# RWKV attention and two MLP layers on one core: gate kept in PSUM, later diagonals, one load for r and k

## The chip, the cores and the metric

The kernel runs on one NeuronCore of one Trainium2 chip. The metric is the device time of one execution in microseconds (us); the median of three runs is 890.35 us. TensorE multiplies, ScalarE evaluates gates and rounds, VectorE and GpSimd do elementwise work, SyncE (SP) issues most DMAs.

## The reference

```python
for t in range(S):                       # B, H, S, D = 4, 8, 768, 48
    kt, vt, rt = k[:, :, t], v[:, :, t], r[:, :, t]
    cur = einsum('bhd,bhe->bhde', u[None] * kt, vt)
    y[:, :, t] = einsum('bhd,bhde->bhe', rt, state + cur)
    state = w[None, :, :, None] * state + einsum('bhd,bhe->bhde', kt, vt)
x = y as (B * S, 384)                    # 3072 tokens
h = x @ w_in; x = (h * sigmoid(1.702 * h)) @ w_out        # 384 -> 2048 -> 384
h = x @ w_in2; out = (h * tanh(softplus(h))) @ w_out2
```

## The kernel before, in words

The sequence is cut into 6 chunks of 128 steps. Chunk by chunk and batch by batch (24 blocks n; batch n % 4) attention is done with matmuls: the scores k·r of all pairs of steps of a chunk (`scores`, two PSUM banks), a mask (VectorE, `select`, line 741), the diagonal with u instead of the decay (`diagonal`: a reduction at 752 and a predicated copy at 757), the product with v (`inside`), the part from the state (`before`) and the new state (`update`, then `add_state`, 775 and 779). r and k are multiplied by powers of the decay first, by VectorE for the first blocks (`decay_half`, `decay_rk`) and by GpSimd later (`prepare`, 471); `bonus` (457, 459) is GpSimd's r*k*u for the diagonal. `decay_k` multiplies k in rows (735 on VectorE).

Each tile of the MLP is one chunk of all four batches, 512 columns. There are 6 tiles in each of the two layers. A tile has 16 units f, each 128 of the 2048 hidden features; in the first tile the first 10 units are done as two halves of 256 columns, so it has 26 steps. All numbers are split in a high part (rounded to TensorE's fp32r) and a low part, and each product is three: high*high, low*high, high*low. So a unit g is `up` (9 matmuls to a bank of h, line 1016), the gate, and `down` (9 matmuls into three accumulators, line 1045). There are 202 units in all and two banks of h. TensorE's order is written out by hand: step g issues up(g+2), with the attention work of the step behind its first matmul, and then down(g). What attention stands in which step is in the tables `SCORES` and `BURST` (first tile: scores of block 2 at step 1, its `inside` at step 3; block 3 at 4 and 6; 4 at 9 and 11; 5 at 12 and 14; 6 at 16 and 18; 7 at 19 and 21).

The gate is evaluated twice by ScalarE from the same bank: once to SBUF in full precision (`act1`, 589), once rounded to `g_hi` (592), which waits until down(g-2) has read the old `g_hi`. VectorE makes `g_lo = act1 - g_hi` (798). up(g) waits for `g_hi` of g-2, since its bank of h is free then. The weights' low parts in the first tile are made by GpSimd (482, 487).

y of a block is rounded to the high part of x by ScalarE (569), its low part is made by VectorE (764); for blocks of later tiles both go to a staging buffer `xt`, and SP moves them in 10 DMAs (`move_x`) to their place in x, `xs`. SP's queue is in the order of its code. r and k of a block come in two DMAs of 48 rows (48 or 64 in the first), to partitions 0 and 64.

At the start TensorE runs matmuls that nothing reads (`keep_warm`, 878; each call makes two instructions), turns the row u into columns (`selector_rows`, 963), and then goes to the scores of block 0. ScalarE copies those columns (617), then reverses the decay table (620), which VectorE needs for the second half of r and k.

The lines around the gate:

```python
act.activation(act1[:, g % 2, 0:c1 - c0], h_bank[g % 2][:, 0:c1 - c0], GATES[layer])
if g >= 2:
    act.wait_ge(g_used, g - 1)
act.activation(g_hi[:, g % 2, 0:c1 - c0], h_bank[g % 2][:, 0:c1 - c0], GATES[layer]).then_inc(g_done, 1)
```

Of the kernel before, what the change touches and what calls it, by code (L numbers as in the profile page):

```python
# [27 lines left out]
P = 128  # L28
CH = P
# [8 lines left out]
MOVES = 10  # L38
AHEAD = 2
BY_ACT = (0, 2)  # L40
WARM = (5, 10)
MID_STEPS = (3, 6, 9)
EARLY = 2
HALF = 10
# [10 lines left out]
def mlp_rwkv_program(nc, rk_d, r_d, k_d, v_d, w_d, u_d, wts_d, out_d):  # L55
# [9 lines left out]
    with ExitStack() as ctx:  # L65
        def sb(name, shape, dt=F32):
            return ctx.enter_context(nc.sbuf_tensor(name, shape, dt))

        def sem(name):
            return ctx.enter_context(nc.semaphore(name))  # L70
# [4 lines left out]
        wout_hi = sb("wout_hi", [P, NF, DM], F32R)  # L75
        wout_lo = sb("wout_lo", [P, NF, DM], F32R)
        xs = sb("xs", [P, 2, 2 * KD, TT], F32R)
        xt = sb("xt", [P, 2, HP, CH], F32R)
        mid = sb("mid", [P, NT * KD * TT])
        g_hi = sb("g_hi", [P, 2, TT], F32R)  # L80
        g_lo = sb("g_lo", [P, 2, TT], F32R)
        act1 = sb("act1", [P, 2, TT])


        ARENA = 9168
# [3 lines left out]
        def part(cols):  # L89
            place[0] += cols  # L90
            assert place[0] <= ARENA
            return arena[:, place[0] - cols:place[0]]
# [3 lines left out]
        mask = part(CH)  # L96
        ident = part(P)

        rk = [part(2 * HP * CH)[0:PR_ROWS, :].rearrange("p (a h t) -> p a h t", a=2, h=HP) for _ in range(2)]
        ks = [part(DM).rearrange("p (h d) -> p h d", h=H) for _ in range(2)]  # L100
        vs, rr = [part(DM).rearrange("p (h d) -> p h d", h=H)], [part(DM)]
        late = part(2 * DM)
# [30 lines left out]
        def first_operands(b):  # L133

            e = operands(b)
            if b == 0:
                e.amat = act1.rearrange("p a t -> p (a t)").rearrange("p (a h t) -> p a h t", a=2, h=HP)
            if b < EARLY:
                e.ks = held[b].rearrange("p (h d) -> p h d", h=H)
                e.vs = held[EARLY + b].rearrange("p (h d) -> p h d", h=H)  # L140
            return e
# [68 lines left out]
        win_ready, wout_ready = sem("win_ready"), sem("wout_ready")  # L210
        wout_first = sem("wout_first")
        h_done = sem("h_done")
        g_done = sem("g_done")
        glo_done = sem("glo_done")
        g_used = sem("g_used")
# [20 lines left out]

            return slot(f)[:, DM:2 * DM]

        def rk_rows(n):

            return ODD if n < EARLY else D

        def rk_half(n, j):

            rows = rk_d[bass.ds(n, 1)].rearrange("o j d a h t -> (o j d) a h t")
            return rows[D:2 * D] if j else rows[0:rk_rows(n)]

        def x_pieces(n):

            a, b = divmod(n, B)  # L250
            par = a % 2
            cols = slice(b * CH, (b + 1) * CH)
            for head in range(H):
                hp, half = divmod(head, 2)
                done = 0
                while done < D:
                    kd, q = divmod(head * D + done, P)
                    m = min(D - done, P - q)
                    q0 = hp % 2 * ODD + done
                    yield f32(xs[q:q + m, :, par * KD + kd, cols]), f32(xt[q0:q0 + m, :, half * 2 + hp // 2, :])  # L260
                    done += m

        def x_part(lo, par, kd):
# [9 lines left out]
        def x_block(lo, n):  # L273

            b = n % B
            if n < B:
                return xs[:, lo, 0:KD, b * CH:(b + 1) * CH]
            return xt[0:PR_ROWS, lo].rearrange("p (a i) t -> p a i t", a=2)

        def y_block(n):  # L280

# [53 lines left out]
        @block.sync  # L335
        def _(sp):
            def load_rk(n):
                sp.dma_start(buffers(n).rk[0:rk_rows(n)], rk_half(n, 0)).then_inc(rk_in[n % B], 16)
                if n >= EARLY:
                    sp.dma_start(buffers(n).rk[ODD:PR_ROWS], rk_half(n, 1)).then_inc(rk_in[n % B], 16)  # L340

            def load_k(n):
                sp.dma_start(buffers(n).ks, k_d[bass.ds(n, 1)].rearrange("o t h d -> t (o h) d")).then_inc(k_first[n] if n < EARLY else k_in[n % B], 16)
# [70 lines left out]
            for n in range(B, NT * B):  # L414
                if n + 2 < NT * B:
                    sp.wait_ge(y_done, n + 1)
                    load_rk(n + 2)
                move_x(n)
                if n + 2 < NT * B:
                    load_rest(n + 2)  # L420

            sp.wait_ge(xlo_done, NT * B)
# [14 lines left out]
        def _(pool):  # L437
# [28 lines left out]
            def prepare(n):  # L466

                a, b = divmod(n, B)
                e = buffers(n)
                pool.wait_ge(rk_in[b], a * 32 + 32)  # L470
                pool.tensor_tensor(e.rk, e.rk, decay, ALU.mult).then_inc(r_dec, 1)  # L471

            def rest(n):
# [69 lines left out]
        def _(act):  # L543
# [20 lines left out]
            def x_hi_part(n):  # L564

                act.wait_ge(y_done, n + 1)
                if n > B:
                    act.wait_ge(moved[(n - 1) % B], moves(n - 1))
                act.activation(x_block(0, n), y_block(n), ACT.Copy).then_inc(xhi_done, 1)

            def first_state(n):
# [11 lines left out]
            def gate(layer, g):  # L583

                f, c0, c1 = unit(g)
                act.wait_ge(h_done, g + 1)
                if g >= 2:
                    act.wait_ge(glo_done, g - 1)
                act.activation(act1[:, g % 2, 0:c1 - c0], h_bank[g % 2][:, 0:c1 - c0], GATES[layer])  # L589
                if g >= 2:  # L590
                    act.wait_ge(g_used, g - 1)
                act.activation(g_hi[:, g % 2, 0:c1 - c0], h_bank[g % 2][:, 0:c1 - c0], GATES[layer]).then_inc(g_done, 1)  # L592

            def copy_out(layer, t):

# [12 lines left out]
            act.wait_ge(cleared, 1)  # L608
            act.dma_start(powers[ODD:PR_ROWS, 0, 0, :], w_d[1]).then_inc(w_in, 16)
            act.dma_start(u_row, u_d).then_inc(u_first, 16)  # L610
            for n in range(EARLY):
                act.dma_start(first[n].rk[ODD:PR_ROWS], rk_half(n, 1)).then_inc(rk_in[n], 16)
            act.preload_act_table(GATES[0])
            act.wait_ge(cleared, 2)
            act.wait_ge(pick_rows, 1)
            for p0 in (0, ODD):
                act.activation(pick[p0:p0 + D, :], decay_bank[p0:p0 + D, 0:HP], ACT.Copy).then_inc(pick_copied, 1)

            act.wait_ge(runs, LOGS)
            act.activation(decay[:, 1], decay[:, 0, :, ::-1], ACT.Copy).then_inc(flipped, 1)  # L620
# [65 lines left out]
        def _(dve):  # L686
# [19 lines left out]

            def decay_half(n, a):

                dve.wait_ge(rk_in[n], 32)
                dve.tensor_tensor(first[n].rk[:, a], first[n].rk[:, a], decay[:, a], ALU.mult).then_inc(r_first, 1)  # L710

            def decay_rk(n):

                dve.wait_ge(rk_in[n], 32)
                dve.tensor_tensor(first[n].rk, first[n].rk, decay, ALU.mult).then_inc(r_first, 1)

            def split(win, wout):
# [63 lines left out]
            def attention(t, s):  # L781

                if s in SCORES[t]:
                    select(SCORES[t][s])
                    diagonal(SCORES[t][s])
                if s in BURST[t]:
                    x_lo_part(BURST[t][s])
                    if B <= BURST[t][s] < (NT - 1) * B:
                        add_state(BURST[t][s])

            def split_g(g):

                f, c0, c1 = unit(g)
                cols = slice(0, c1 - c0)
                dve.wait_ge(g_done, g + 1)
                if g >= 2:
                    dve.wait_ge(g_used, g - 1)
                dve.tensor_tensor(g_lo[:, g % 2, cols], act1[:, g % 2, cols], f32(g_hi[:, g % 2, cols]), ALU.subtract).then_inc(glo_done, 1)  # L798

            def split_mid(par, tile, kd):  # L800

# [65 lines left out]
        def _(pe):  # L867
# [89 lines left out]
            def selector_rows():  # L957

                pe.wait_ge(u_first, 16)
                for hp in range(HP):  # L960
                    for half, p0 in enumerate((0, ODD)):
                        d0 = (2 * hp + half) * D
                        ins = pe.matmul(decay_bank[p0:p0 + D, hp:hp + 1], u_row[:, d0:d0 + D], ident[0:1, 0:1], start=True, stop=True)
                ins.then_inc(pick_rows, 1)

            def early_sums(n):
# [26 lines left out]
            def up(g, beside):  # L993

                t, (f, c0, c1) = tile_of(g), unit(g)
                layer = t // NT
                par = t % 2
                hb = h_bank[g % 2][:, 0:c1 - c0]
                pe.wait_ge(win_ready, layer * NF + f + 1)
                if g >= 2:  # L1000
                    pe.wait_ge(g_done, g - 1)
                if f == 0 and layer:
                    pe.wait_ge(m_hi, (t - NT) * KD + KD)
                elif f == 0:
                    for b in range(c0 // CH, c1 // CH):
                        if t:
                            pe.wait_ge(moved[b], moves(t * B + b))
                        else:
                            pe.wait_ge(xhi_done, b + 1)
                for i, (w, lo) in enumerate(((win_hi, 0), (win_lo, 0), (win_hi, 1))):  # L1010
                    if f == 0 and lo and layer:
                        pe.wait_ge(m_lo, (t - NT) * KD + KD)
                    elif f == 0 and lo and t == 0:
                        pe.wait_ge(xlo_done, c1 // CH)
                    for kd in range(KD):
                        ins = pe.matmul(hb, w[:, f, kd, :], x_part(lo, par, kd)[:, c0:c1], start=i + kd == 0, stop=i == 2 and kd == KD - 1)  # L1016
                        if i == 2 and kd == KD - 1:
                            ins.then_inc(h_done, 1)
                        if i + kd == 0:
                            beside()  # L1020
# [105 lines left out]
```

## Time and profile before

| what | value |
|---|---|
| three runs | 889.5, 890.35, 891.91 us |
| the profiled execution | 891.0 us, its span 889.2 us |
| TensorE busy | 882.1 us, 99% |
| VectorE busy | 328.7 us, 37% |
| ScalarE busy | 292.5 us, 33% |
| GpSimd busy | 156.4 us, 18% |
| mean granted clock of TensorE | 0.998 of full speed |

Busy TensorE is time in which at least one matmul was in flight. The chain that ended last goes through TensorE for 96% of the span. In a timeline row, "x3" are three instructions run together, and what is in brackets is the engine's idle time before the first one and what released it.

### The profile page before, as it was taken

The page shows a single profiled execution, that of the slowest core. Times are in us where ns is not written, and L with a number is a line of the kernel's source. Part 1 is how long each engine was busy: PE and PEld are TensorE (multiplying, and loading weights), DVE is VectorE, ACT ScalarE, POOL GpSimd, SP SyncE. Part 2 cuts the span into 40 slices and gives each one's busy share as a digit, 9 for nine tenths or more (in the row PEclk, how much of TensorE's full clock was granted, in tenths as well). Part 3 has the DMA queues.
Part 4 walks back from the last instruction along what each step waited for, and adds up shares of the span by engine and source line. Part 5 has one row for each costly group of instructions (what it writes and reads, how often), then busy time and mean ns, then how long its engine had stood idle before and what let it go on. Part 6 is the DMA issues. An engine that isn't in the chain of part 4 may idle for free.

```text
span 889.2 us, 12953 instructions
## 1 busy us (share of the span) xinstructions
PE 882.1 (99%) x5168; PEld 730.6 (82%) x5168; DVE 328.7 (37%) x460; ACT 292.5 (33%) x540; POOL 156.4 (18%) x126
## 2 busy tenths in 40 slices
PE   9999999999999999999999999999999999999998
PEld 8998888887888878878888888888888888888886
DVE  6878336424443443543244222222222221221111
ACT  4542332232223222222454422322322322322322
POOL 5998403322231331120000000000000000000000
PEclk9999999999999999999999999999999999999999
DMA  9554303212330332221430000000000000000000
GB/s 248 170 170 118 95 25 97 83 48 63 88 99 12 86 93 63 51 77 38 157 107 18 1 0 1 36 1 1 35 1 1 36 1 1 35 1 1 36 1 35
DMA packets 37836, 49.54 MB, mean 56 GB/s; under 512 B 5873, under 2 KB 30322, under 8 KB 37778
## 3 DMA queue, kind: packets, MB, share of 16 engines
q1 hardware_dynamic: 37120, 48.13, 18.2%
q8 instruction: 42, 0.69, 0.3%
q10 hardware_dynamic: 658, 0.59, 0.3%
q14 instruction: 16, 0.13, 0.0%
HBM read 36.11 MB, written 4.72 MB: 46 GB/s over the span
## 4 chain that ended last, share of the span: by engine, by line
PE 96%; POOL 1%; DVE 1%; issue 1%; ACT 0%; POOLq 0%; DVEq 0%
PE h L1016 44%; PE acc L1045 43%; PE a_bank L895 2%; PE pair L928 2%; PE pair L941 1%; PE a_bank L953 1%; PE acc L878 1%; POOL win_lo L482 0%; POOL wout_lo L487 0%; DVE g_lo L798 0%; PE pair L878 0%; POOL arena L457 0%; PE h L895 0%; PE pair L914 0%; PE pair L921 0%
## 5 line engine op out<-in xcount | busy, mean ns | idle before, releaser
L798 DVE TENSOR_TENSOR g_lo<-act,g_hi 128x512 fp32r<-128x512 f32 (+1 forms) x202 | 173.1, 858 | 507.0 <-ACT g_hi L592 506.8
L1016 PE MATMUL h<-xs,win_hi 128*128 128x512 f32 (+1 forms) x1212 | 340.6, 384 | 0.2 <-POOL win_lo L482 0.2
L1016 PEld LDWEIGHTS h<-xs,win_hi 128*128 128x128 f32 x1212 | 220.2, 188 | 45.1 <-issue 0.7
L589 ACT ACTIVATE act<-h 128x512 f32<-128x512 f32 (+1 forms) x202 | 116.4, 576 | 268.9 <-PE h L1016 266.0
L592 ACT ACTIVATE g_hi<-h 128x512 fp32r<-128x512 f32 (+1 forms) x202 | 116.5, 577 | 254.4 <-PE acc L1045 254.3
L1045 PE MATMUL acc<-g_hi,wout_hi 128*128 128x512 f32 (+1 forms) x606 | 168.1, 379 | 0.0
L1045 PE MATMUL acc<-g_hi,wout_lo 128*128 128x512 f32 (+1 forms) x606 | 167.8, 379 | 0.0
L1045 PE MATMUL acc<-g_lo,wout_hi 128*128 128x512 f32 (+1 forms) x606 | 167.6, 378 | 0.0
L1016 PE MATMUL h<-xs,win_lo 128*128 128x512 f32 (+1 forms) x606 | 164.8, 380 | 0.0
L1045 PEld LDWEIGHTS acc<-g_hi,wout_hi 128*128 128x128 f32 x606 | 111.6, 189 | 21.8
L1016 PEld LDWEIGHTS h<-xs,win_lo 128*128 128x128 f32 x606 | 111.2, 188 | 22.0
L1045 PEld LDWEIGHTS acc<-g_hi,wout_lo 128*128 128x128 f32 x606 | 111.4, 189 | 21.3
L1045 PEld LDWEIGHTS acc<-g_lo,wout_hi 128*128 128x128 f32 x606 | 111.1, 188 | 21.3
L471 POOL TENSOR_TENSOR arena<-arena 112x1024 f32<-112x1024 f32 x20 | 48.7, 2437 | 129.7 <-DMA arena<-in_rk 129.7
L457 POOL TENSOR_TENSOR arena<-arena 128x384 f32<-128x384 f32 x22 | 24.4, 1110 | 99.0 <-DMA arena<-in_r 98.6
L757 DVE COPY_PREDICATED arena<-arena 128x1024 f32<-128x1024 uint32 x22 | 30.8, 1402 | 0.8
L895 PEld LDWEIGHTS a_bank<-arena 48*128 48x128 f32 x184 | 22.2, 187 | 8.1 <-issue 7.4
L895 PE MATMUL a_bank<-arena 48*128 48x128 f32 x184 | 26.4, 284 | 1.5 <-DVE arena L779 1.5
L895 PE MATMUL pair<-arena 48*128 48x128 f32 x184 | 26.5, 284 | 0.0
L606 ACT ACTIVATE mid<-acc 128x512 f32<-128x512 f32 x24 | 14.3, 598 | 33.8 <-PE acc L1045 33.8
L459 POOL TENSOR_TENSOR arena<-arena 128x384 f32<-128x384 f32 x22 | 23.4, 1063 | 1.7
L895 PEld LDWEIGHTS pair<-arena 48*128 48x128 f32 x184 | 22.2, 187 | 0.0
(92 smaller groups left out, 373.3 us busy)
## 6 DMA issues: line engine op xcount, KB each, us to landing
arena<-in_rk SPq DMA_DIRECT2D x44, 192.0 KB, 3.3
mid<-in_wts SPq DMA_DIRECT2D x16, 384.0 KB, 7.8
arena<-in_wts SPq DMA_DIRECT2D x16, 384.0 KB, 3.5
xs<-xt SPq DMA_DIRECT2D x117, 48.0 KB, 2.0
arena<-in_k SPq DMA_DIRECT2D x22, 192.0 KB, 2.6
arena<-in_r SPq DMA_DIRECT2D x22, 192.0 KB, 3.1
arena<-in_v SPq DMA_DIRECT2D x22, 192.0 KB, 2.7
out<-mid SPq DMA_DIRECT2D x5, 768.0 KB, 3.3
```

The lines of the kernel that those rows point to most:

```text
L457: pool.tensor_tensor(heads, heads, e.ks, ALU.mult).then_inc(rr_step, 1)
L459: pool.tensor_tensor(e.rr, e.rr, bonus_u, ALU.mult).then_inc(rr_step, 1)
L471: pool.tensor_tensor(e.rk, e.rk, decay, ALU.mult).then_inc(r_dec, 1)
L589: act.activation(act1[:, g % 2, 0:c1 - c0], h_bank[g % 2][:, 0:c1 - c0], GATES[layer])
L592: act.activation(g_hi[:, g % 2, 0:c1 - c0], h_bank[g % 2][:, 0:c1 - c0], GATES[layer]).then_inc(g_done, 1)
L606: act.activation(mid_cols(t - layer * NT, kd), acc[kd][:, :], ACT.Copy).then_inc(out_done[kd], 1)
L757: dve.copy_predicated(buffers(n).amat, ident.bitcast(mybir.dt.uint32).rearrange("p (a h t) -> p a h t", a=1, h=1).broadcast_to([P, 2, HP, ...
L798: dve.tensor_tensor(g_lo[:, g % 2, cols], act1[:, g % 2, cols], f32(g_hi[:, g % 2, cols]), ALU.subtract).then_inc(glo_done, 1)
L895: ins = pe.matmul(banks[half][:, hp * CH:(hp + 1) * CH], e.rk[p0:p0 + D, 1, hp, :], e.rk[p0:p0 + D, 0, hp, :], start=True, stop=True)
L928: ins = pe.matmul(y_part(n, hp, half), e.vs[:, 2 * hp + half, :], e.amat[:, half, hp, :], start=n < B and i == 0, stop=i == 1, skip_group_ ...
L1016: ins = pe.matmul(hb, w[:, f, kd, :], x_part(lo, par, kd)[:, c0:c1], start=i + kd == 0, stop=i == 2 and kd == KD - 1)
L1045: ins = pe.matmul(acc[kd][:, c0:c1], w[:, f, kd * P:(kd + 1) * P], lo[:, g % 2, 0:c1 - c0], start=i == 0 and opens, stop=i == 2 and ends, ...
```

## The change

ScalarE's gate writes over h in its bank, and `g_hi` is a rounding copy of the result; VectorE subtracts `g_hi` from the bank, and up(g) waits for `g_lo` of g-2. `act1` is gone. `xt` has two buffers. In the first tile `diagonal` of a block comes one step after `select`. r and k of a block come in one DMA of 128 rows (two for the last block); k, v and r of a block after the next are asked for before the moves of x, except behind each fourth block. The matmuls that turn u have 128 columns instead of one, and there are 4 and 6 calls of `keep_warm` around them instead of 5 and 10.

```diff
-WARM = (5, 10)
+WARM = (4, 6)
-        xt = sb("xt", [P, 2, HP, CH], F32R)
+        xt = sb("xt", [P, 2, 2, HP, CH], F32R)
...
@@ block.sync, load_rk @@
-                sp.dma_start(buffers(n).rk[0:rk_rows(n)], rk_half(n, 0)).then_inc(rk_in[n % B], 16)
-                if n >= EARLY:
-                    sp.dma_start(buffers(n).rk[ODD:PR_ROWS], rk_half(n, 1)).then_inc(rk_in[n % B], 16)
+                cols = 2 * HP * CH
+                if n + 1 < NT * B:
+                    halves = bass.AP(tensor=rk_d.tensor, offset=n * 2 * D * cols, ap=[[D * cols, 2], [cols, ODD], [1, cols]])
+                    sp.dma_start(rk_rows[n % 2], halves).then_inc(rk_in[n % B], 16)
...
@@ block.sync, the loop over blocks @@
                     load_rk(n + 2)
+                    if n % B < B - 1:
+                        load_rest(n + 2)
                 move_x(n)
-                if n + 2 < NT * B:
+                if n + 2 < NT * B and n % B == B - 1:
                     load_rest(n + 2)
...
@@ ScalarE, x_hi_part @@
-                if n > B:
-                    act.wait_ge(moved[(n - 1) % B], moves(n - 1))
+                if n > B + 1:
+                    act.wait_ge(moved[(n - 2) % B], moves(n - 2))
...
@@ ScalarE, gate; h_cols(g) is h_bank[g % 2][:, 0:c1 - c0] @@
                 act.wait_ge(h_done, g + 1)
-                if g >= 2:
-                    act.wait_ge(glo_done, g - 1)
-                act.activation(act1[:, g % 2, 0:c1 - c0], h_bank[g % 2][:, 0:c1 - c0], GATES[layer])
+                act.activation(h_cols(g), h_cols(g), GATES[layer]).then_inc(g_full, 1)
                 if g >= 2:
                     act.wait_ge(g_used, g - 1)
-                act.activation(g_hi[:, g % 2, 0:c1 - c0], h_bank[g % 2][:, 0:c1 - c0], GATES[layer]).then_inc(g_done, 1)
+                act.wait_ge(g_full, g + 1)
+                act.activation(g_hi[:, g % 2, 0:c1 - c0], h_cols(g), ACT.Copy).then_inc(g_done, 1)
...
@@ ScalarE, start: issues of DMAs and copy of u's columns @@
-            for n in range(EARLY):
-                act.dma_start(first[n].rk[ODD:PR_ROWS], rk_half(n, 1)).then_inc(rk_in[n], 16)
...
-                act.activation(pick[p0:p0 + D, :], decay_bank[p0:p0 + D, 0:HP], ACT.Copy).then_inc(pick_copied, 1)
+                act.activation(pick[p0:p0 + D, :], decay_bank[p0:p0 + D, 0:HP * P:P], ACT.Copy).then_inc(pick_copied, 1)
...
@@ VectorE, attention @@
                 if s in SCORES[t]:
                     select(SCORES[t][s])
+                if t and s in SCORES[t]:
                     diagonal(SCORES[t][s])
+                if t == 0 and s - 1 in SCORES[t]:
+                    diagonal(SCORES[t][s - 1])
...
@@ VectorE, split_g @@
-                dve.tensor_tensor(g_lo[:, g % 2, cols], act1[:, g % 2, cols], f32(g_hi[:, g % 2, cols]), ALU.subtract).then_inc(glo_done, 1)
+                dve.tensor_tensor(g_lo[:, g % 2, cols], h_cols(g), f32(g_hi[:, g % 2, cols]), ALU.subtract).then_inc(glo_done, 1)
...
@@ TensorE, selector_rows @@
-                        ins = pe.matmul(decay_bank[p0:p0 + D, hp:hp + 1], u_row[:, d0:d0 + D], ident[0:1, 0:1], start=True, stop=True)
+                        ins = pe.matmul(decay_bank[p0:p0 + D, hp * P:(hp + 1) * P], u_row[:, d0:d0 + D], ident[0:1, :], start=True, stop=True)
...
@@ TensorE, up @@
                 if g >= 2:
-                    pe.wait_ge(g_done, g - 1)
+                    pe.wait_ge(glo_done, g - 1)
```

## Rows read from the trace of the kernel before

**Rows 1.** The page, part 1: busy us, share of the span, instructions.

```profile
PE 882.1 (99%) x5168; PEld 730.6 (82%) x5168; DVE 328.7 (37%) x460; ACT 292.5 (33%) x540; POOL 156.4 (18%) x126
```

**Rows 2.** TensorE's waits: total us, times, longest us.

```profile
PE a_bank L895 <- DVE arena L779: 1.5, 1, 1.5
PE h L1016 <- POOL win_lo L482: 0.2, 1, 0.2
```

**Rows 3.** Timeline, a late step: start us, us, instruction, [idle before].

```profile
836.99 0.60 ACT L592 ACTIVATE g_hi<-h 128x512 fp32r<-128x512 f32 x1 [1.44 <-PE acc L1045]
837.62 0.69 DVE L798 TENSOR_TENSOR g_lo<-act,g_hi 128x512 fp32r<-128x512 f32 x1 [3.39 <-ACT g_hi L592]
838.83 0.39 PE L1045 MATMUL acc<-g_hi,wout_hi 128*128 128x512 f32 x1
```

**Rows 4.** Timeline, TensorE, 77 to 90 us.

```profile
77.37 0.39 PE L1016 MATMUL h<-xs,win_hi 128*128 128x512 f32 x1
...
79.65 0.73 PE L1016 MATMUL h<-xs,win_hi 128*128 128x512 f32 x2
...
82.67 0.39 PE L1016 MATMUL h<-xs,win_hi 128*128 128x512 f32 x1
84.54 0.34 PE L895 MATMUL a_bank<-arena 48*128 48x128 f32 x1 [1.47 <-DVE arena L779]
...
85.63 0.73 PE L1016 MATMUL h<-xs,win_hi 128*128 128x512 f32 x2
...
90.19 0.87 PE L1016 MATMUL h<-xs,win_hi 128*128 128x512 f32 x3
```

**Rows 5.** Busy time by window: us, PE, PEld, DVE, ACT, POOL, granted clock, DMA.

```profile
85.60:90.20 4.60, 4.60 (x20) 3.90 (x19) 3.94 (x4) 0.60 (x1) 2.90 (x2) 0.63 0.22 55
```

**Rows 6.** Timeline, VectorE, 76 to 84 us.

```profile
76.18 5.48 DVE L798 TENSOR_TENSOR g_lo<-act,g_hi 128x256 fp32r<-128x256 f32 x1
...
83.93 0.35 DVE L779 TENSOR_TENSOR arena<-arena,a_bank 112x192 f32<-112x192 f32 x1
```

**Rows 7.** By line, 20 to 96 us: ns min/median/max; L752: whole span, mean last.

```profile
L741 DVE TENSOR_TENSOR arena<-a_bank,arena x6: 676/690/692, 25.4 to 85.7; 128x512 f32<-128x512 f32 x6
...
L798 DVE TENSOR_TENSOR g_lo<-act,g_hi x23: 408/1162/5483, 21.5 to 95.2; 128x256 fp32r<-128x256 f32 x20, 128x512 fp32r<-128x512 f32 x3
...
L757 DVE COPY_PREDICATED arena<-arena x6: 1329/1425/2185, 27.2 to 87.5; 128x1024 f32<-128x1024 uint32 x6
...
L752 DVE TENSOR_REDUCE arena<-arena 128x8 f32<-128x384 f32 x22 | 11.9, 540 | 0.0
```

**Rows 8.** Timeline, GpSimd, 75 to 81 us.

```profile
74.97 3.53 POOL L471 TENSOR_TENSOR arena<-arena 112x1024 f32<-112x1024 f32 x1
...
80.37 1.01 POOL L482 TENSOR_TENSOR win_lo<-mid,win_hi 128x384 fp32r<-128x384 f32 x1
```

**Rows 9.** Timeline, the first units.

```profile
21.06 0.38 ACT L592 ACTIVATE g_hi<-h 128x256 fp32r<-128x256 f32 x1
...
21.29 0.89 PE L1016 MATMUL h<-xs,win_hi 128*128 128x256 f32 x6
```

**Rows 10.** Timeline, units 3 to 5 and block 2.

```profile
27.45 0.38 ACT L592 ACTIVATE g_hi<-h 128x256 fp32r<-128x256 f32 x1 [0.70 <-PE acc L1045]
...
29.62 0.88 PE L914 MATMUL pair<-arena 128*64 128x128 f32 x12
```

**Rows 11.** Timeline, the start.

```profile
4.46 0.80 PE L963 MATMUL acc<-arena 1*48 1x1 f32 x16
5.20 4.64 PE L878 MATMUL acc<-arena 128*128 128x128 f32 x20
...
6.22 0.63 ACT L620 ACTIVATE arena<-arena 112x512 f32<-112x512 f32 x1 [0.47 <-DVE arena L703]
...
9.77 1.84 PE L895 MATMUL h<-arena 48*128 48x128 f32 x16
...
11.71 1.29 DVE L741 TENSOR_TENSOR act<-h,arena 128x512 f32<-128x512 f32 x2 [1.22 <-PE h L895]
```

More of the change, by code:

```diff
@@ L81, in mlp_rwkv_program @@
         g_lo = sb("g_lo", [P, 2, TT], F32R)
-        act1 = sb("act1", [P, 2, TT])
         ARENA = 9168
@@ L97, in mlp_rwkv_program @@
         ident = part(P)
-        rk = [part(2 * HP * CH)[0:PR_ROWS, :].rearrange("p (a h t) -> p a h t", a=2, h=HP) for _ in range(2)]
+        rk_rows = [part(2 * HP * CH) for _ in range(2)]
+        rk = [rows[0:PR_ROWS, :].rearrange("p (a h t) -> p a h t", a=2, h=HP) for rows in rk_rows]
         ks = [part(DM).rearrange("p (h d) -> p h d", h=H) for _ in range(2)]
@@ L136, in first_operands @@
             if b == 0:
-                e.amat = act1.rearrange("p a t -> p (a t)").rearrange("p (a h t) -> p a h t", a=2, h=HP)
+                e.amat = xt[:, 1].bitcast(F32)
             if b < EARLY:
@@ L212, in mlp_rwkv_program @@
         h_done = sem("h_done")
+        g_full = sem("g_full")
         g_done = sem("g_done")
@@ L237, in staged_out, with h_cols @@
             return slot(f)[:, DM:2 * DM]
[L239 to L246, printed above, removed]
+        def h_cols(g):
+            f, c0, c1 = unit(g)
+            return h_bank[g % 2][:, 0:c1 - c0]
         def x_pieces(n):
@@ L259, in x_pieces @@
                     q0 = hp % 2 * ODD + done
-                    yield f32(xs[q:q + m, :, par * KD + kd, cols]), f32(xt[q0:q0 + m, :, half * 2 + hp // 2, :])
+                    yield f32(xs[q:q + m, :, par * KD + kd, cols]), f32(xt[q0:q0 + m, n % 2, :, half * 2 + hp // 2, :])
                     done += m
@@ L277, in x_block @@
                 return xs[:, lo, 0:KD, b * CH:(b + 1) * CH]
-            return xt[0:PR_ROWS, lo].rearrange("p (a i) t -> p a i t", a=2)
+            return xt[0:PR_ROWS, n % 2, lo].rearrange("p (a i) t -> p a i t", a=2)
         def y_block(n):
@@ L337, in load_rk @@
             def load_rk(n):
-                sp.dma_start(buffers(n).rk[0:rk_rows(n)], rk_half(n, 0)).then_inc(rk_in[n % B], 16)
-                if n >= EARLY:
-                    sp.dma_start(buffers(n).rk[ODD:PR_ROWS], rk_half(n, 1)).then_inc(rk_in[n % B], 16)
+                cols = 2 * HP * CH
+                if n + 1 < NT * B:
+                    halves = bass.AP(tensor=rk_d.tensor, offset=n * 2 * D * cols, ap=[[D * cols, 2], [cols, ODD], [1, cols]])
+                    sp.dma_start(rk_rows[n % 2], halves).then_inc(rk_in[n % B], 16)
+                else:
+                    for j in range(2):
+                        sp.dma_start(rk_rows[n % 2][j * ODD:j * ODD + D, :],
+                                     rk_d[n, j].rearrange("d a h t -> d (a h t)")).then_inc(rk_in[n % B], 16)
             def load_k(n):
@@ L469, in prepare @@
                 e = buffers(n)
-                pool.wait_ge(rk_in[b], a * 32 + 32)
+                pool.wait_ge(rk_in[b], a * 16 + (16 if n + 1 < NT * B else 32))
                 pool.tensor_tensor(e.rk, e.rk, decay, ALU.mult).then_inc(r_dec, 1)
@@ L707, in decay_half @@
             def decay_half(n, a):
-                dve.wait_ge(rk_in[n], 32)
+                dve.wait_ge(rk_in[n], 16)
                 dve.tensor_tensor(first[n].rk[:, a], first[n].rk[:, a], decay[:, a], ALU.mult).then_inc(r_first, 1)
             def decay_rk(n):
-                dve.wait_ge(rk_in[n], 32)
+                dve.wait_ge(rk_in[n], 16)
                 dve.tensor_tensor(first[n].rk, first[n].rk, decay, ALU.mult).then_inc(r_first, 1)
@@ L997, in up @@
                 par = t % 2
-                hb = h_bank[g % 2][:, 0:c1 - c0]
+                hb = h_cols(g)
                 pe.wait_ge(win_ready, layer * NF + f + 1)
                 if g >= 2:
-                    pe.wait_ge(g_done, g - 1)
+                    pe.wait_ge(glo_done, g - 1)
                 if f == 0 and layer:
```

## The prediction, on record before the result was known

> **What bounds the kernel.** I read the page's busy shares first: TensorE is busy 99% of the span [rows 1], so the other engines count only where they make it wait or lower its clock. Then its waits: apart from the 2.0 us before its first instruction there are two, 1.5 us for VectorE's addition to the state (L779) and 0.2 us for GpSimd's `win_lo` [rows 2]. So nothing done to ScalarE's gate or VectorE's split in the other stages can be worth anything unless it delays TensorE. In a step of the second layer the reader sees the room: `g_hi` starts at 836.99, `g_lo` runs 837.62 to 838.31, and the next up product begins 2.04 us after the down product at 838.83, at 840.87 [rows 3]. A unit's `g_lo` is 2.56 us ahead of the product that will overwrite its bank of h.
>
> The one costly place lies in the first tile (19.4 to 94 us), where TensorE waits before the scores of block 7. An up product starts at 82.67 and the score matmuls only at 84.54; the same pair stands 0.32 us apart where nothing is late, so 1.55 us are lost. The stretch behind it (8 wide up matmuls, 9 half-width down ones) takes 85.63 to 90.19, 4.56 us, where the same set took 79.65 to 82.67, 3.02 us [rows 4]: another 1.54 us, because the granted clock averages 0.63 in that stretch, that is, mostly the lower level (1.2 of 2.4 GHz), right behind the idle time [rows 5]. Together **3.1 us**. Its cause is VectorE's queue: one `g_lo` of 256 columns runs from 76.18 for 5.48 us, and its three successors end in L779 at 84.28 [rows 6]. The same instruction takes 0.41 us at its shortest [rows 7]. During it GpSimd ran four tensor_tensors back to back, from the L471 at 74.97 to the L482 at 80.37 [rows 8], and `g_lo` ended 0.3 us behind the last of them. Both inputs of `g_lo` lie in SBUF. Instructions of VectorE with one input in PSUM, in the same crowded stretch, vary by some nanoseconds only: L741 takes 676 to 692 ns for 512 columns, while `g_lo` spreads from 408 to 5483 and L757 from 1329 to 2185 [rows 7].
>
> **Gate in place in PSUM.** ScalarE's work is unchanged in count: 202 gates and 202 copies for 404 gates, 0.38 us at 256 columns and 0.60 at 512 [rows 3, 9]. The copy must now wait for the gate's end, which the two overlapped ones didn't; I take 0.1 us. In all units where `g_hi` is held back by a down product anyway (836.99 is such a place) that is hidden. What changes is `g_lo`: its first input moves to PSUM, so by the L741 row it takes 0.41 (256) or 0.69 us (512) whatever GpSimd does. So the 5.48 us instruction becomes 0.41, L779 ends ahead of TensorE's need even with the moved diagonal (about 82 for 82.99), and the 3.1 us go: **-3.1**; 0, if it blocks as before. GpSimd, no longer held off by `g_lo`, delivers `win_lo` sooner: **-0.2** for the second wait [rows 2]; at least 0.
>
> The price is that the up product of unit g+2 now waits for `g_lo` of g (before: for `g_hi`). In full-width units the 2.56 us of room covers it, 0 cost in 182 of 202 units. In the first units it doesn't. `g_hi` of unit 0 runs 21.06 to 21.44; the third up product begins at 21.65, the fourth of six matmuls 0.12 apart in the row at 21.29 [rows 9]. With 0.14 us for the serialised copy, `g_lo` runs 21.62 to 22.03, so TensorE is held **+0.4** (0.3 to 0.6). For the other half-width units `g_hi` is early enough: unit 3's ends at 27.83, and unit 5's up product begins one matmul before 29.62, at 29.41 [rows 10], so a free `g_lo` has 1.2 us to spare. The cover is a short queue on VectorE. If that is gone it costs the difference; the worst of the trace of before is the `g_lo` of unit 18, which ended at 81.66 where unit 20's up product had begun at 77.37 [rows 4, 6]: 4.3 us, the high end.
>
> **Diagonals moved one step later in tile 0.** This is the part that can hurt. `g_lo` goes in front of the tensor_reduce and the predicated copy, and nothing else is between them and TensorE's `inside(n)`, which needs them. For block 2: `g_hi` of unit 3 ends at 27.83 [rows 10], held until then by a down product. Behind it `g_lo` 0.41, reduce 0.54, copy 1.33 [rows 7], with 0.04 between instructions: the diagonal is ready at 30.24. TensorE wants it at 29.62 [rows 10]: late by 0.6, and the decay of k in front of it (SBUF inputs, blocked by GpSimd in the trace of before) may add 0.2. Block 3 has the same pattern: 0.6 without the addition. Both also carry the copy's median excess of 0.1 over its shortest. Since everything from the down product's end shifts with TensorE, the lateness isn't absorbed. Sum **+1.4** for both; bounds: 0.8, if instructions overlap by 0.1 each, and 3.1 with the copy at its worst. Blocks 4, 5 and 6 have 16 state matmuls (0.58 us) before the need, which makes clean copies just in time: **+0.3** for the three (0 to 2.4, three times 0.8 at the copy's worst; I go by its median). Block 7 stands among full-width units and has room.
>
> **Start of the kernel.** Ten warm-up instructions fewer (5+10 calls of two instructions become 4+6), each 0.23 us (20 in 4.64): -2.3. But the 16 instructions that turn u, 0.80 us with one column, get 128 columns, and then cost as the warm-up's, 16 x 0.23 = 3.7: +2.9. TensorE alone would reach the scores of block 0 0.6 later than 9.77 [rows 11]. Also the selector is ready at about 7.7 instead of 5.3 and ScalarE copies it before it reverses the decay table, whose reversal at 6.22 took 0.63 and now ends at about 8.7; VectorE needs it for r and k (0.6 us for each of three halves, so 10.6, or about 11.9 with GpSimd's product in between). That is covered as long as VectorE can start its masks at 11.71 [rows 11]; from there to the first up product VectorE is the chain. Against it stands the clock: the 16 score matmuls of block 0 took 1.84 us from 9.77, the 16 at 84.54 1.09, so the clock rose only about 11.3, and ahead of it lay the near-empty 0.80 us of narrow products [rows 4, 11]. With full products there the clock may rise earlier and the scores end up to 1 us sooner; if it rises when it did, they end up to 0.5 later. **-0.2**, from -1.0 to +0.5.
>
> **r and k in one DMA.** One issue on SP's queue for two (on ScalarE's, none for two), 128 rows for 112. GpSimd's waits for r in the attention stages shrink, since k, v and r of a block now stand ahead of the ten moves of x on SP's queue; the moves start three issues later, are needed only by the next tile, and the fourth block's keep their place. TensorE waits for none of this: 0. Two buffers for y remove a wait of ScalarE that no row shows as the last: 0.
>
> **Sum.** -3.1 -0.2 +0.4 +1.4 +0.3 -0.2 = -1.4 us on the profiled execution's 891.0 (span 889.2, and 1.8 around it): 889.6. That execution lies 0.65 above the median of the three (890.35), which may be part of the stall; I take **889.3** for the median.
>
> The Trainium skill (SBUF — State Buffer, section Who interferes with whom) says that a VectorE instruction with two SBUF inputs and a GpSimd one that reads SBUF block each other fully, the second until the first finishes. The trace disagrees in the length: this `g_lo` was held through four GpSimd instructions. By the rule as written it would have ended about 78.9 and there would be no stall to remove.
>
> **Rivals.** (A) *More comes back.* The stall goes whole, diagonals are on time to 0.1 us except the first two, and the clock rises early: -3.3 +0.4 +0.9 -0.8 = -2.8, on the median near 887.5. For it: VectorE's spreads collapse. Against it: the arithmetic of 29.62. (B) *The stall isn't in the median.* A 5.48 us hold is one event; if the other executions (889.5 the lowest) have it shorter, there is nothing to remove, and only the new waits are left: 890.35 +2.1 -0.2 = about 892.2. For it: the other `g_lo` of the stretch have a median of 1162 ns. (C) *The diagonal takes the stall's place* (the one on the other side): inside(2) to inside(6) wait at the copy's worst, 3.1 + 2.4, and one of them lowers the clock again, 1.5: 891.0 -3.3 +0.4 +5.5 +1.5 -0.2 = 894.9. It decides once the diagonals' waits, with the clock behind them, pass 3.1 us together. For it: half of the copies' six durations are above 1.42, and one is 2.19 [rows 7]. Against it: it takes nearly every copy at its worst. (D) *`g_lo` still blocks*: the wait on it binds at unit 20 (+4.3) and the clock falls behind it, with the old stall kept and the diagonals' price: 891.0 +4.3 +2.1 = about 897. L741's row speaks against it.
>
> **Numbers.** Forecast 0.47 (its own range 888 to 891), A 0.27, B 0.15, C 0.08, D 0.03. A run of this kernel tells 0.3%, 2.7 us, from nothing. Faster by that (under 887.7): over half of A and the edge of the forecast, 0.26. Slower (over 893.0): C, D and an edge of B, 0.12. Same: 0.62. The range 886.6 to 892.5 leaves out C, D and the ends.
>
> **What would show it.** `g_lo` at 0.41 and 0.69 us everywhere; no wait for L779 and no low clock behind the start; a short wait before the third up product; waits of TensorE at inside(2) and inside(3) for the predicated copy, 0.5 to 0.8 each; steps of 2.04 us per nine matmuls unchanged. A `g_lo` from PSUM over 1 us, or more than 1 us at one diagonal, would make it wrong.

## The result: 952.7 us, 7% slower

| | median us | runs |
|---|---|---|
| before | 890.7 | 4 |
| changed | 952.69 (951.36 to 953.74) | 4 |

The ratio is 1.0695, with a 95% interval of 1.0675 to 1.0715: 62 us slower, where 889.3 was forecast and 886.6 to 892.5 given as the range. The profiled execution took 952.65 us, its span is 950.9.

The page of the changed kernel, beside [rows 1]: TensorE's busy time grew by 14 us (its mean granted clock is 0.98 instead of 0.998), the rest of the 62 is idle.

```profile
PE 895.9 (94%) x5158; PEld 739.5 (78%) x5158; DVE 294.6 (31%) x460; ACT 291.1 (31%) x540; POOL 145.9 (15%) x126
...
PE 82%; DMA 9%; SPq 6%; ACT 1%; DVE 1%; issue 1%; POOL 0%; ACTq 0%; DVEq 0%; POOLq 0%
```

The second line is the chain that ended last: DMAs and SP's queue hold 15% of it. TensorE's waits, beside [rows 2] (total us, times, longest):

```profile
PE h L1020 <- DMA xs<-xt: 13.1, 4, 3.4
PE a_bank L899 <- DVE arena L711: 9.3, 1, 9.3
PE pair L918 <- ACT arena L634: 9.1, 1, 9.1
PE h L899 <- DVE arena L711: 8.2, 1, 8.2
PE h L1020 <- DVE g_lo L802: 5.0, 3, 2.6
```

L711 is the decay of r and k of blocks 0 and 1, L634 the padding of v: both stand behind loads. L1020 is an up product at the start of a tile, which waits for the moves of x. SP's queue and VectorE in the start (timeline of the changed kernel: start us, us, instruction, idle before it and what ended that):

```profile
2.69 8.75 SPq L348 DMA_DIRECT2D mid<-in_v  x2
...
15.66 1.29 DVE L711 TENSOR_TENSOR arena<-arena 112x512 f32<-112x512 f32 x2 [9.47 <-DMA arena<-in_rk]
```

r and k of block 0, asked for at 1.36, have all landed at 15.5 instead of 6.6. And SP, which issued the two loads of v in 1.06 us before, now needs 8.75: its queue is held up behind the load in front. The page's DMA issues show it for the whole kernel (KB each, median us from issue to landing; in the kernel before k, v and r took 2.6, 2.7 and 3.1 and these moves of x 2.0):

```profile
xs<-xt SPq DMA_DIRECT2D x117, 48.0 KB, 3.1
arena<-in_k SPq DMA_DIRECT2D x22, 192.0 KB, 13.0
arena<-in_r SPq DMA_DIRECT2D x22, 192.0 KB, 12.9
arena<-in_v SPq DMA_DIRECT2D x22, 192.0 KB, 13.0
```

Busy time by window says why (the last two numbers are the mean busy share of the 16 DMA engines and GB/s); first the changed kernel from 4 to 10 us, when only loads of r and k are under way:

```profile
4.00:10.00 6.00, 4.84 (x29) 4.11 (x28) 1.96 (x10) 1.48 (x4) 0.20 (x1) 1.00 0.13 51
```

then the kernel before from 4 to 9 us:

```profile
4.00:9.00 5.00, 5.00 (x37) 4.76 (x37) 3.32 (x13) 1.52 (x5) 1.27 (x2) 1.00 1.04 232
```

A share of 0.13 is 2 of 16. The load's source pattern is `[[D * cols, 2], [cols, 64], [1, cols]]`: an outermost dimension of 2, and two engines carry 64 rows each. A row of 4096 bytes takes an engine 0.159 us in the trace (median of the packets), 64 of them 10.2 us, and two engines at that rate move 51.5 GB/s, the 51 of the row. The load's semaphore, which counts to 16, shows it too: 14 of its counts come at once, two some 12 us later (77.7 and 78.5 for a load issued at 64.83). Two counts are late for the loads behind it as well: of the load of k issued at 65.64, 14 counts come from 67.7 to 68.0 and the last two at 78.2 and 79.0. The Trainium skill has this rule (DMA: Bandwidth & Descriptors, section Why a DMA increments its semaphore by 16 and not by 1): a DMA uses the largest number of engines up to 16 that divides the slowest dimension of both patterns. Every number above agrees with it.

Where the 62 us accrue: the first up product starts at 38.1 instead of 19.4 (+18.7), that of tile 1 at 152.7 instead of 108.8 (+43.9), and tiles 2, 3, 4 and 5 begin 50.3, 56.4, 59.9 and 61.7 late. From there, with no blocks left to load, nothing is added.

### The profile page after: what moved, and what is told of

Same layout as the page of the kernel before. It is cut to its first block, busy times and chain, and to the rows that moved or that the text cites. A ratio compares the mean times of both kernels' runs of the same rounds, so it can differ in the third digit from the quotient of the medians.

```text
span 950.9 us, 12909 instructions
## 1 busy us (share of the span) xinstructions
PE 895.9 (94%) x5158; PEld 739.5 (78%) x5158; DVE 294.6 (31%) x460; ACT 291.1 (31%) x540; POOL 145.9 (15%) x126
## 4 chain that ended last, share of the span: by engine, by line
PE 82%; DMA 9%; SPq 6%; ACT 1%; DVE 1%; issue 1%; POOL 0%; ACTq 0%; DVEq 0%; POOLq 0%
PE h L1020 39%; PE acc L1049 37%; DMA xs<-xt 4%; DMA mid<-in_wts 4%; PE a_bank L899 2%; PE pair L932 2%; SPq L364 2%; DMA arena<-in_rk 2%; SPq L345 1%; SPq L348 1%; PE pair L945 1%; SPq L372 1%; SPq L338 1%; PE a_bank L957 0%; DVE xt L765 0%
## 5 line engine op out<-in xcount | busy, mean ns | idle before, releaser
L1020 PE MATMUL h<-xs,win_hi 128*128 128x512 f32 (+1 forms) x1212 | 345.5, 388 | 18.1 <-DMA xs<-xt 13.1
L802 DVE TENSOR_TENSOR g_lo<-h,g_hi 128x512 fp32r<-128x512 f32 (+1 forms) x202 | 134.3, 665 | 557.6 <-ACT g_hi L595 557.6
L1020 PEld LDWEIGHTS h<-xs,win_hi 128*128 128x128 f32 x1212 | 222.9, 191 | 65.4 <-issue 21.3
L591 ACT ACTIVATE h<-h 128x512 f32<-128x512 f32 (+1 forms) x202 | 113.4, 562 | 286.9 <-PE h L1020 284.1
L1020 PE MATMUL h<-xs,win_lo 128*128 128x512 f32 (+1 forms) x606 | 166.8, 384 | 0.0
L1020 PEld LDWEIGHTS h<-xs,win_lo 128*128 128x128 f32 x606 | 112.9, 192 | 22.3
L899 PE MATMUL a_bank<-arena 48*128 48x128 f32 x184 | 29.0, 302 | 12.2 <-DVE arena L711 9.3
L899 PEld LDWEIGHTS a_bank<-arena 48*128 48x128 f32 x184 | 24.3, 203 | 19.3 <-DVE arena L711 9.6
L899 PE MATMUL pair<-arena 48*128 48x128 f32 x184 | 29.0, 302 | 0.0
L899 PEld LDWEIGHTS pair<-arena 48*128 48x128 f32 x184 | 24.3, 203 | 0.0
```

The lines of the kernel that those rows point to most:

```text
L591: act.activation(h_cols(g), h_cols(g), GATES[layer]).then_inc(g_full, 1)
L802: dve.tensor_tensor(g_lo[:, g % 2, cols], h_cols(g), f32(g_hi[:, g % 2, cols]), ALU.subtract).then_inc(glo_done, 1)
L899: ins = pe.matmul(banks[half][:, hp * CH:(hp + 1) * CH], e.rk[p0:p0 + D, 1, hp, :], e.rk[p0:p0 + D, 0, hp, :], start=True, stop=True)
```

## The experiments

**The load alone, four ways.** e1_two_loads, for the same 128 rows:

```diff
                 cols = 2 * HP * CH
-                if n + 1 < NT * B:
-                    halves = bass.AP(tensor=rk_d.tensor, offset=n * 2 * D * cols, ap=[[D * cols, 2], [cols, ODD], [1, cols]])
-                    sp.dma_start(rk_rows[n % 2], halves).then_inc(rk_in[n % B], 16)
...
+                for j in range(2):
+                    rows = ODD if n + 1 < NT * B else D
+                    half = bass.AP(tensor=rk_d.tensor, offset=(n * 2 + j) * D * cols, ap=[[cols, rows], [1, cols]])
+                    sp.dma_start(rk_rows[n % 2][j * ODD:j * ODD + rows, :], half).then_inc(rk_in[n % B], 16)
```

> The changed kernel, but each 128-row load of r and k is issued as two DMAs of 64 rows (one row per entry of the outermost dimension), same bytes to the same places. Theory E (the load's access pattern has an outermost dimension of 2, so its data goes over 2 of the 16 DMA engines: two late increments per load, some 12 us from issue to landing): loads land in 2 to 5 us again, the waits for r and k go, first up product near 19.5 us, time 889.3 (887 to 892), what was forecast for the rest of the change. Rival S (the size: 14% more rows are read, and across the border to the next half): 930 or more. Rival G (the gate in PSUM and the later diagonals are part of the +62): 895 to 930.

e2_one_load_padded, with the array padded in DRAM to 128 rows a block (it replaces all of `load_rk`):

```diff
+                sp.dma_start(rk_rows[n % 2], rk_d[n].rearrange("p a h t -> p (a h t)")).then_inc(rk_in[n % B], 16)
```

> The changed kernel with r and k laid out in DRAM in 128 rows per block (16 rows of zeros behind each 48), so that one DMA of 128 rows has an outermost dimension of 128. Theory E: as with two loads, within 1 us: one DMA isn't slow by being one. Rival O (one DMA of 512 KB is slower than two, whatever its pattern): 940 or more.

e3_51_rows, as e1 with

```diff
-                    rows = ODD if n + 1 < NT * B else D
+                    rows = ODD if n < EARLY else 51 if n + 1 < NT * B else D
```

> As with two loads, but from block 2 on each half has 51 rows (the last three unused) where the kernel before had 48; blocks 0 and 1 have 64. 51 is 3 x 17. Theory E in its general form (the engines used are the largest number up to 16 that divides the rows): 3 engines, so 13 increments come at once and 3 late, 102 rows x 0.159 us / 3 = 5.4 us a block and a landing after 6 to 7; the start is undisturbed (first up near 19.5), then some 10 us are lost in tiles 0 to 4: 900 (893 to 915). Rival S: fewer bytes than 64 rows, so as with two loads, 889.3.

e4_before_one_load is the kernel before with the change's `load_rk` (and the buffers of 128 rows and the counts that it needs; as in the change, ScalarE issues no part of the first loads).

> The kernel before with nothing changed but the load of r and k, which is the change's single DMA (two entries of 64 rows). Theory E: it alone costs what the change cost plus what the rest gains, 890.4 + 62 = 952 (945 to 962). Rival G: 910 to 940, the rest of the change being part of the loss.

| kernel | engines by the rule | median us (4 runs each) | ratio to before, interval |
|---|---|---|---|
| changed | 2 | 952.69 | 1.0695, 1.0675 to 1.0715 |
| e4_before_one_load | 2 | 953.74 | 1.0717, 1.0699 to 1.0736 |
| e3_51_rows | 3 (block 2 on) | 902.5 | 1.0143, 1.0128 to 1.0158 |
| e1_two_loads | 16 | 894.32 | 1.0047, 1.0032 to 1.0062 |
| e2_one_load_padded | 16 | 893.43 | 1.0042, 1.0025 to 1.0059 |

The ratio of the changed kernel is to the 890.7 above, the others to 889.5, the median of the seven runs of the kernel before that were made beside them. Theory E holds in all four as to the cause. Splitting the pattern takes off 58 us; one DMA of 512 KB is as good as two if its outermost dimension is 128; 51 rows are slower than 64; and the load alone, put in the kernel before, costs 64 us. S (the size) and O (one DMA slower than two) fall. E's times came out for e2, e3 and e4, but not for e1: 894.32 lies above its 887 to 892, by what the rest of the change costs (below). The window of e1, same columns as above:

```profile
4.00:9.00 5.00, 5.00 (x31) 4.34 (x32) 4.02 (x13) 1.71 (x6) 1.53 (x2) 1.00 1.04 262
```

In e3's trace each load of 51 rows has three late counts on its semaphore, not two or sixteen. In the profiles its loss against e1 is the expected 10 us (8.2 between the medians), but it stands whole at the start of tile 1 (10.6 us, 10.7 at tile 2) and isn't spread over tiles 0 to 4.

What is left is a loss of 4.8 us in e1 and 3.9 in e2, where the forecast had a gain of 1.4. The profiled executions show only 1.8 and 1.0 of it, all of it before tile 1. In e1's profile TensorE's waits are (total, times, longest; the 2.0 before its first instruction left out):

```profile
PE pair L929 <- DVE arena L755: 3.5, 3, 2.7
...
PE pair L915 <- DVE arena L755: 1.8, 2, 1.3
PE h L1017 <- DVE g_lo L799: 0.4, 1, 0.4
```

L755 is the diagonal's predicated copy. So TensorE waits 5.3 us for the later diagonals there, and 2.7 in e2's profile. Neither profile is of a typical execution, though: both have a mean clock of 1.0, while three of e1's four executions and two of e2's have 0.998 and are 1.3 to 2.4 us longer than the profiled one. No kept trace shows where the clock falls in those.

**The parts, one by one.** The four kernels of this group ran on another chip than e1 and e2, each beside runs of the kernel before. f1_diag_at_once is e2 with

```diff
-                if t and s in SCORES[t]:
                     diagonal(SCORES[t][s])
-                if t == 0 and s - 1 in SCORES[t]:
-                    diagonal(SCORES[t][s - 1])
```

> The changed kernel with the padded load (893.4 median), and the diagonal of a block in the first tile right behind its mask again. Theory D (the later diagonal is what TensorE waits for: 2.7 us of waits for the predicated copy in that kernel's profile, 5.3 in the one with two loads): those waits go; in their place g_lo of units 3 and 6 stands behind a diagonal and a decay of k and is late for the up products of units 5 and 8 by 0.8 and 0.6. Net -1.3: 892.1 (890.5 to 893). Rival B (the start, not the diagonals, is what the rest of the change loses): unchanged, 893.4 within 0.7.

f2_decay_k_later is f1 with

```diff
-                    if t == 0 and s == 1:
+                    if t == 0 and s == 2:
                         dve.wait_ge(dtab, 2)
                         decay_k(2)
-                    if t == 0 and s == 2:
                         decay_rk(3)
-                    if t == 0 and s == 4:
+                    if t == 0 and s == 5:
                         decay_k(3)
```

> As f1_diag_at_once, and the decay of k of blocks 2 and 3 one step later, behind g_lo, where its product needs it only 2 us after. Theory D: both kinds of wait go, -2.7 against 893.4: 890.7 (889 to 892), in the profile no wait of TensorE for VectorE over 0.5. Rival B: 893.4.

f3_before_gate_in_psum is the kernel before with the change's hunks in `gate`, `split_g` and `up` alone.

> The kernel before with only the gate evaluated once in place in PSUM, g_hi a rounding copy, g_lo from PSUM and its bank released by g_lo. My forecast's terms: g_lo 0.42 and 0.69 us throughout, the wait before the scores of block 7 and the low clock behind it gone (-3.1 on the profiled execution, less on the median if it is not in every execution), +0.4 at the third up product, +1.4 for g_lo of units 3 and 6: 888.5 (887 to 891) against 889.5. Rival: g_lo as a release costs in all full-width units or the in-place gate is slower: 893 or more.

f4_start_as_before is e2 with `WARM = (5, 10)` and the one-column products.

> The changed kernel with the padded load (893.4), and the start as before: u turned by one column, 5 and 10 warm-up calls. My forecast had -0.2 for the new start, from -1.0 to +0.5: here 893.6 (892.9 to 894.4). Rival B (the start is where the rest of the change loses, since the clock of that profile rose only at 15.0 and the first up product stood at 20.5 instead of 19.4): 891.5 or less.

| kernel | median us (runs) | ratio to before (889.96, 28 runs), interval |
|---|---|---|
| f1_diag_at_once | 889.32 (12) | 0.9996, 0.9984 to 1.0009 |
| f2_decay_k_later | 888.14 (7) | 0.9977, 0.9967 to 0.9988 |
| f3_before_gate_in_psum | 893.09 (8) | 1.0029, 1.0019 to 1.0038 |
| f4_start_as_before | 894.26 (12) | 1.0033, 1.0021 to 1.0045 |

Theory D: undoing the later diagonal gives back 4.1 us (0.46% by the ratios), more than was expected, and moving the decay of k another 1.2, which the intervals hardly separate (TensorE's waits for `g_lo` go from 2.2 to 1.0 us). Both times lie under the ranges that were expected for them. Part of the 4.1 goes with the clock. f4 has the later diagonals too: ten of its twelve executions have a mean clock of 0.996 to 0.998 and a median of 894.4, the two with 1.0 took 890.8 and 889.8. Of f1's twelve, one has so low a clock. So late diagonals go together with a low clock in most executions; that they cause it isn't shown, for the profiles of e1, e2 and f4 are all of executions without it. The start is neutral: f4's median is 0.8 us above e2's and its ratio 0.0009 below, each against its own runs of before, and the intervals overlap. The rival of its expectation falls. The start also varies by itself: with the same start code the first up product comes at 18.7 us in e1's profile and at 20.5 in e2's, where the clock rises at 10.8 and at 15.0. The gate in PSUM alone was forecast as a gain and is a loss of 3.1; its time is that of the rival (893 or more), but not for the rival's reasons. Its profile has the `g_lo` that was promised,

```profile
L803 DVE TENSOR_TENSOR g_lo<-h,g_hi 128x512 fp32r<-128x512 f32 x182 | 125.8, 691 | 516.9 <-ACT g_hi L597 516.9
L803 DVE TENSOR_TENSOR g_lo<-h,g_hi 128x256 fp32r<-128x256 f32 x20 | 8.3, 418 | 16.6 <-ACT g_hi L597 16.6
```

691 and 418 ns on average, where both forms were held before (821 and 1193 in the kernel before); and yet TensorE waits for it:

```profile
PE h L1021 <- DVE g_lo L803: 3.5, 3, 2.0
```

That is three waits in 202 units, not one in each. The longest comes from the instruction in front of `g_lo` in VectorE's queue:

```profile
75.26 4.08 DVE L762 COPY_PREDICATED arena<-arena 128x1024 f32<-128x1024 uint32 x1
79.25 0.73 DVE L803 TENSOR_TENSOR g_lo<-h,g_hi 128x256 fp32r<-128x256 f32 x2
```

The hold of [rows 6] has not gone. It has moved to the copy in front of `g_lo`, which has all its operands in SBUF: the copy took 1.33 us there before, and starts now 1.4 us behind GpSimd's decay of r and k (`prepare`, 73.86) instead of just ahead of it. Behind TensorE's wait the granted clock is 0.50 from 80.3 to 83.7 us, and all eight executions of f3 have a mean clock of 0.996 to 0.998.

**Does the order of the loads count, and can the load stay unpadded?** g1_two_loads_repaired is f2 with e1's load; g2_old_load_order is f2 with

```diff
                     load_rk(n + 2)
-                    if n % B < B - 1:
-                        load_rest(n + 2)
                 move_x(n)
-                if n + 2 < NT * B and n % B == B - 1:
+                if n + 2 < NT * B:
                     load_rest(n + 2)
```

> f2_decay_k_later with the load as two DMAs of 64 rows from the unpadded array instead of one from the padded one. Theory E: each uses all 16 engines, so the way the rows are packed is worth no more than between the two kernels measured first (894.3 and 893.4): 888.1 to 889.3. Rival: one issue instead of two is what keeps SP's queue ahead, 890.5 or more.

> f2_decay_k_later with k, v and r of a block asked for behind the moves of x again, as in the kernel before. My forecast priced this part at 0, since TensorE waits for none of it: 888.1 within 0.7. Rival (GpSimd's later products of r, k and u hold VectorE's copies longer, or the diagonal waits for r): 889.5 or more.

| kernel | median us (runs) | ratio to before (890.99, 23 runs), interval |
|---|---|---|
| g1_two_loads_repaired | 894.81 (12) | 1.0045, 1.0032 to 1.0058 |
| g2_old_load_order | 890.48 (11) | 1.0000, 0.9988 to 1.0012 |

Both miss: g1 by over 5 us, g2 by about 2, and both times are those of the rivals. But g1's profile doesn't show the rival's reason, SP's queue. VectorE:

```profile
62.44 5.76 DVE L755 COPY_PREDICATED arena<-arena 128x1024 f32<-128x1024 uint32 x1
68.10 0.73 DVE L796 TENSOR_TENSOR g_lo<-h,g_hi 128x256 fp32r<-128x256 f32 x2
```

GpSimd in the same stretch:

```profile
61.77 2.40 POOL L472 TENSOR_TENSOR arena<-arena 112x1024 f32<-112x1024 f32 x1 [3.70 <-DMA arena<-in_rk]
64.13 1.01 POOL L483 TENSOR_TENSOR win_lo<-mid,win_hi 128x384 fp32r<-128x384 f32 x1
65.10 0.99 POOL L488 TENSOR_TENSOR wout_lo<-mid,wout_hi 128x384 fp32r<-128x384 f32 x1
66.06 0.99 POOL L483 TENSOR_TENSOR win_lo<-mid,win_hi 128x384 fp32r<-128x384 f32 x1
67.01 2.02 POOL L488 TENSOR_TENSOR wout_lo<-mid,wout_hi 128x384 fp32r<-128x384 f32 x1
```

The copy waits through four of GpSimd's instructions, one of them under way when it starts, and gets in before the fifth, which is 1 us longer than its fellows for it. In f2 the same row of GpSimd begins at 59.92 instead of 61.77, since GpSimd waits less long for r and k, and the copy of that block takes 1.62 us. TensorE waits for the `g_lo` behind, and its clock falls (a wait, and a window of 9 us with the granted clock in the third column from the right):

```profile
68.65 0.55 PE L1013 MATMUL h<-xs,win_hi 128*128 128x256 f32 x1 [3.63 <-DVE g_lo L796]
```

```profile
66.00:75.00 9.00, 6.35 (x61) 5.68 (x62) 4.14 (x6) 1.05 (x3) 5.93 (x6) 0.62 0.23 62
```

**Is it GpSimd's unbroken row of instructions?** h1_two_loads_gpsimd_pauses (on g1) and h2_best_gpsimd_pauses (on f2) both have

```diff
             prepare(6)
+            pool.wait_ge(diag_done, 6)
             low(12, 14)
             rest(6)
             prepare(7)
+            pool.wait_ge(diag_done, 7)
             low(14, NF)
```

> g1_two_loads_repaired (894.8; its predicated copy of block 5 took 5.76 us) with two waits on GpSimd: behind the decay of r and k of blocks 6 and 7 it waits for the diagonal of blocks 5 and 6 before it goes on with the weights' low parts. Theory H (VectorE's instruction with two SBUF inputs is held as long as GpSimd has instructions back to back, and gets in only where GpSimd is late): the copy is held for the rest of one instruction, at most 3.7 us and mostly under 3, the 3.6 us wait for g_lo and the low clock behind it (about 2 to 3) shrink or go: 889.5 (888 to 891.5). Rival W (the two loads themselves make the difference of 6.7 us to the padded one, by what they do to SP's queue or the DMA engines): 894 to 895.

> f2_decay_k_later (888.14; its copies took 1.62, 2.78 and 1.52 us in tile 0) with the same two waits on GpSimd. Theory H: little left to gain, 887.9 (887 to 888.6), and its executions spread less. Rival: the weights' low parts come later and hold TensorE's up products, 889.5 or more.

| kernel | median us (12 runs each) | ratio to before (891.37, 23 runs), interval |
|---|---|---|
| h1_two_loads_gpsimd_pauses | 888.81 | 0.9979, 0.9968 to 0.9990 |
| h2_best_gpsimd_pauses | 888.28 | 0.9965, 0.9951 to 0.9979 |

h1 against g1: 6.0 us less for two waits. VectorE's copy and GpSimd in h1:

```profile
62.32 2.81 DVE L757 COPY_PREDICATED arena<-arena 128x1024 f32<-128x1024 uint32 x1
```

```profile
61.54 2.42 POOL L472 TENSOR_TENSOR arena<-arena 112x1024 f32<-112x1024 f32 x1 [3.57 <-DMA arena<-in_rk]
65.20 1.01 POOL L483 TENSOR_TENSOR win_lo<-mid,win_hi 128x384 fp32r<-128x384 f32 x1 [1.25 <-DVE arena L757]
```

The copy is held for the rest of one instruction. W falls: the two loads cost nothing by themselves that these runs can tell, they shift GpSimd's row under the copy. The clock goes with it: ten of g1's twelve executions have a mean clock of 0.996 to 0.998, none of h1's. h2 has the lowest ratio to before, 0.35% under it; TensorE's only wait for VectorE in its profile is the one of 0.4 at the third up product. Its gain over f2 can't be told: 888.28 and 888.14, from different chips. That its executions would spread less did not come true (3.1 us from lowest to highest, 2.5 in f2).

## Why the prediction was wrong

The step that failed is **r and k in one DMA**, priced at 0: "TensorE waits for none of this". I counted issues and rows, 128 for 112, and took for granted that the transfer would spread as before. The source pattern's outermost 2 was in the diff. It made the load about 14 us long or longer, held up SP's issues, and delayed the last two counts of the loads behind it, so TensorE did wait. e4 measures that term at +64 us where I had 0, with no bound at all; none of the rivals was about it.

With the load repaired the forecast would still have been too low (893.4 and 894.3 for 889.3, range up to 892.5). Nearest to it is rival C, the diagonal in the stall's place, which I gave 0.08: 894.9, from 5.5 us of waits at the diagonals and a low clock behind one of them. e1's profile has 5.3 us of such waits; e2's has 2.7. The other steps:

- **The stall before block 7** (-3.1). That VectorE is held while GpSimd has instructions back to back was read rightly, its removal wrongly. `g_lo` is free (418 ns, forecast 410), and in no profile with a repaired load does TensorE wait for L779 (for `win_lo`, the -0.2, only in g1, 0.5 us). But the diagonal's copy is held instead: 4.08 us in f3, 4.09 in e1, 5.76 in g1. Nor were the 3.1 us in every execution: of the 23 of the kernel before beside g1, 13 have a mean clock of 0.996 to 0.998 (median 891.32) and ten one of 1.0 (median 889.76), so the clock's part, 1.5 us, is missing in nearly half of them. Rival B had this half right. (Behind the held `g_lo` stand four instructions up to the end of L779, not three; the 84.28 stands.)
- **Release by `g_lo`** at the third up product: +0.4 forecast, 0.4 measured in e1, e2 and h2. In f3 TensorE waits 3.5 us for the same release, because the queue in front of `g_lo` is long. I had priced that (up to 4.3 us) as the case in which the cover is gone, and left it out of the sum.
- **Later diagonals**: +1.7 forecast, 4.1 measured (e2 to f1). Blocks 2 and 3 were late by 0.49 and 1.27 us in e1 (0.6 each forecast, 0.7 with the copy's excess), blocks 4 to 6 by 3.5 together, where I had 0.3. The mis-sized term is the copy, taken at its median of 1.43 from [rows 7], which took 2.18 us on average in e1's tile 0, with one of 4.09. e2's profile, with 0.6 for blocks 4 to 6, shows how much this varies. The rest of the 4.1 may be the low clock of most executions that were not profiled, which I had priced only in rival C; that isn't shown.
- **The start**: -0.2 forecast; f4 and e2 can't be told apart.
- **Order of the loads**: 0 forecast; g2 against f2 says 2.3 us, on different chips, and against their own before 0.23%. That part isn't shown to be free. g2's profile points to GpSimd's phase again, the rival of its expectation: `bonus` waits for r until 69.11 (67.21 in f2), the decay of r and k behind it starts at 72.12 instead of 70.26, and the copy at 73.71 takes 3.92 us (2.78 in f2), behind which TensorE waits 1.8 us for `g_lo`. That this makes the whole difference isn't shown; it wasn't tried with the pauses.

On the rule that I set against the trace: the Trainium skill (SBUF — State Buffer, section Who interferes with whom) has the second instruction wait until the first finishes. The traces of g1 and h1 show that this is too short where GpSimd issues without a gap: in g1 the copy waited through the instruction under way and the next three, in h1 through one. What decides who is next wasn't measured.

## What to carry to other kernels

Read the outermost dimension of a DMA's access patterns before anything else: here the merging of two transfers into one left 2 engines of 16. Where VectorE and GpSimd work in the same stretch, an instruction of VectorE with both inputs in SBUF can be held through several of GpSimd's (four, 5.76 us, in g1); freeing one kind of instruction left the hold to another (f3), while a pause of GpSimd at the right place cut it to the rest of one instruction (2.81 us in h1). One profile is one execution: where the clock of the others differs from its own, it isn't the typical one. And a wait that releases a buffer should not stand behind an engine's fullest queue.

## What was not expected of the hardware

A DMA on two engines slowed those that use all 16: SP needed 7.66 us to issue a load of v that had taken about 0.5, and k, v and r landed 13 us after issue instead of 3. An in-place gate, PSUM to PSUM, took 562 ns on average against 576 to SBUF (583 and 598 at 512 columns). And two waits added to an engine that was not on the chain made the kernel 6.0 us faster.
